# Channel attention and a SiLU feed-forward in fp32: factor sums of batch two moved to VectorE in step 0 and reloaded from DRAM, step 0 reordered, own tiles for step 0's outputs

## The chip, the cores and the metric

One core of one Trainium2 chip. The number is the device time of one execution in microseconds, for the kernel before as the median of 3 runs. A profile is of one execution of its own.

## The reference, cut to what matters

```python
def _attn_ref(q, k, v, tau):            # (2, 6016, 256) each
    qn = q / (np.linalg.norm(q, axis=1, keepdims=True) + 1e-06)
    kn = k / (np.linalg.norm(k, axis=1, keepdims=True) + 1e-06)
    s = kn.transpose(0, 2, 1) @ qn / tau            # 256 x 256 per batch
    s = s - s.max(-1, keepdims=True)
    a = np.exp(s)
    a /= a.sum(-1, keepdims=True) + 1e-09
    return v @ a

def _moe_ref(x, w_in, w_out):           # x (12032, 256), w_in (256, 2048)
    h = x @ w_in
    g = h * (1.0 / (1.0 + np.exp(-h)))
    return g @ w_out
```

## The kernel before, in words

A first stage (to about 97 us) reads q and k, forms the 256 x 256 attention matrix of both batches and folds each into w_in, so that each batch has its own first-layer weight (`wp_raw[b]`). What is left is silu(v @ folded weight) @ w_out over 12032 tokens, in fp32 written as a high and a low fp32r part: each product is three matmuls (high by high, high by low, low by high). Both layers are done in 2x2 blocks with seven products in place of eight (a Strassen form). The seven weight factors of the first layer are three raw blocks (A12, A22, A11) and four sums (S1 to S4). They are called `a_hi`/`a_lo` here.

The tokens go through in 12 steps (6 for each batch, the last of each narrow, 448 columns in place of 512), and a step goes through 8 pairs of blocks of the hidden dimension. A period n is one pair of one step, n = 8 * step + pair, 96 in all. TensorE does in each the seven products p1 ... p7 of the first layer (lines 823 to 825, 21 matmuls), and the second layer for the period before. In step 0 (periods 0 to 7) that second layer is the plain one of eight products (24 matmuls, `output`, lines 870 to 874), and the Strassen one (21 matmuls, lines 883 to 885, weights from the double buffer `ring`, loaded from `s_dram`) takes over at period 9. While step 0 runs, the eight "parts" of the second layer's factors are made: SyncE loads w_out, GpSimd makes sums and high parts (`part`), VectorE the low parts (`split_part`), SyncE stores to `s_dram`. Parts 4 to 7 share one tile, `late_parts`, so that part i+1 is loaded only when part i is stored.

Each engine's order is written out by hand, in program order, with semaphores between the engines. In a period VectorE's two adds make_c22 (line 1558) and make_c21 (line 1567) stand on the chain of that period: the product p7 ends, make_c22 adds, ScalarE applies SiLU and rounds, VectorE subtracts to the low part (`split_h`, line 1572), and TensorE reads it in the next period. Everything else of VectorE is fitted around it.

At the switch of batches (periods 40 to 55) the first-layer factors of batch two take the places of batch one's, pair by pair. In the kernel before, SyncE reloads the raw blocks (`load_a1`), GpSimd makes four sums with six subtractions and two casts (`prepare_a1`), VectorE makes the low parts (`split_a1`, lines 1546 and 1548):

```python
        reload_at = {SWITCH + 1 + 3 * pair // 2 + pair // 6: pair for pair in range(PAIRS)}
```

The tokens of a step (`load_x`, 6 DMAs on SyncE's queue, then 5 adding DMAs on GpSimd's) go through the tile `x_raw`, rounded by ScalarE (`round_x`) and split by VectorE (`split_x`). In the kernel before, step 0's four outputs are copied into `x_raw`, stored from there, and only then are the tokens of step 2 loaded:

```python
            store_std_outputs()
            sp.wait_ge(out_stored, 32)
            load_x(2)
```

SyncE's queue around it: ring loads for periods 8 and 9 (the second waits for the end of period 8 on TensorE), store part 5, load part 6, then the lines above.

## Time and profile before

| | us |
|---|---|
| median of 3 runs | 1074.22 (1074.03 to 1078.78) |
| profiled execution | 1070.89 |
| its span | 1069.1 |
| TensorE busy | 1034.2 (97%) |
| VectorE busy | 934.1 (87%) |
| ScalarE busy | 898.7 (84%) |
| GpSimd busy | 297.6 (28%) |

The profile gives one engine's busy time as the union of its instructions. Instructions of one engine overlap a little, so that one of 0.69 us can follow another by 0.60 us. The idle time in front of an instruction is printed in brackets with what ended it. A period starts at the first matmul of p1 (a row of L823).

### The profile page before, as it was taken

The page shows a single profiled execution, that of the slowest core. Times are in us where ns is not written, and L with a number is a line of the kernel's source. Part 1 is how long each engine was busy: PE and PEld are TensorE (multiplying, and loading weights), DVE is VectorE, ACT ScalarE, POOL GpSimd, SP SyncE. Part 2 cuts the span into 40 slices and gives each one's busy share as a digit, 9 for nine tenths or more (in the row PEclk, how much of TensorE's full clock was granted, in tenths as well). Part 3 has the DMA queues.
Part 4 walks back from the last instruction along what each step waited for, and adds up shares of the span by engine and source line. Part 5 has one row for each costly group of instructions (what it writes and reads, how often), then busy time and mean ns, then how long its engine had stood idle before and what let it go on. Part 6 is the DMA issues. An engine that isn't in the chain of part 4 may idle for free.

```text
span 1069.1 us, 15160 instructions
## 1 busy us (share of the span) xinstructions
PE 1034.2 (97%) x4584; PEld 851.6 (80%) x4584; DVE 934.1 (87%) x1307; ACT 898.7 (84%) x1580; POOL 297.6 (28%) x323
## 2 busy tenths in 40 slices
PE   9999998989999999999978999999999999999997
PEld 8987776767888888888867777888888888888886
DVE  6887685689889899899899999899899899899898
ACT  7997676778898998898867788898898898988875
POOL 3695231143120121221273662121121211210100
PEclk9999999999999999999999999999999999999999
DMA  9993421397786885876975885885876876975742
GB/s 358 397 366 89 151 92 66 133 265 176 199 194 152 215 196 135 216 176 148 255 150 143 225 193 124 219 188 132 235 173 152 217 173 147 229 168 130 176 134 88
DMA packets 107921, 197.06 MB, mean 184 GB/s; under 512 B 9424, under 2 KB 42448, under 8 KB 107712
## 3 DMA queue, kind: packets, MB, share of 16 engines
q1 hardware_dynamic: 82720, 150.07, 43.2%
q0 software_dynamic: 24544, 45.17, 25.9%
q8 instruction: 37, 0.61, 0.2%
q10 hardware_dynamic: 576, 0.85, 0.2%
q14 instruction: 44, 0.36, 0.1%
HBM read 145.82 MB, written 50.23 MB: 183 GB/s over the span
## 4 chain that ended last, share of the span: by engine, by line
PE 71%; DVE 6%; ACT 3%; issue 3%; DMA 2%; SPq 1%; DVEq 0%; POOL 0%; ACTq 0%; POOLq 0%
PE ps_h L823 12%; PE ps_h L825 12%; PE ps_h L824 12%; PE ps_o L883 6%; PE ps_o L884 6%; PE ps_o L885 6%; PE ps_h L883 5%; PE ps_h L885 5%; PE ps_h L884 5%; DVE t_raw L1584 1%; DVE g_lo L1572 1%; DMA ring<-s_dram 1%; PE ps_o L870 1%; PE ps_o L872 1%; PE ps_o L874 1%
## 5 line engine op out<-in xcount | busy, mean ns | idle before, releaser
L1572 DVE TENSOR_TENSOR g_lo<-h,g_hi 128x512 fp32r<-128x512 f32 (+1 forms) x296 | 205.4, 696 | 24.5 <-ACT g_hi L1206 23.2
L1206 ACT ACTIVATE g_hi<-h 128x512 fp32r<-128x512 f32 (+1 forms) x296 | 182.5, 620 | 10.2 <-PE ps_h L885 3.8
...
L823 PE MATMUL ps_h<-b_hi,a_hi_mid 128*128 128x512 f32 (+1 forms) x336 | 132.7, 395 | 6.1 <-ACT h L1183 3.1
L825 PE MATMUL ps_h<-b_hi,a_lo_mid 128*128 128x512 f32 (+1 forms) x336 | 130.9, 390 | 0.0
L824 PE MATMUL ps_h<-b_lo,a_hi_mid 128*128 128x512 f32 (+1 forms) x336 | 130.7, 389 | 0.0
L1558 DVE TENSOR_TENSOR h<-ps_h,w 128x512 f32<-128x512 f32 (+1 forms) x96 | 65.2, 679 | 61.5 <-PE ps_h L825 41.7
L883 PE MATMUL ps_h<-g_hi,ring 128*128 128x512 f32 (+1 forms) x264 | 103.7, 393 | 13.5 <-DVE g_lo L1572 7.2
L1606 DVE TENSOR_TENSOR gx_lo<-t_raw,gx_hi 128x1024 fp32r<-128x1024 f32 (+1 forms) x88 | 107.8, 1225 | 0.6 <-ACT gx_hi L1213 0.6
L1584 DVE TENSOR_TENSOR t_raw<-h 128x1024 f32<-128x1024 f32 (+1 forms) x88 | 107.4, 1221 | 0.0
L883 PE MATMUL ps_o<-gx_hi,ring 128*128 128x512 f32 (+1 forms) x264 | 102.2, 387 | 0.7 <-DVE gx_lo L1616 0.4
L885 PE MATMUL ps_h<-g_hi,ring 128*128 128x512 f32 (+1 forms) x264 | 102.7, 389 | 0.0
L884 PE MATMUL ps_h<-g_lo,ring 128*128 128x512 f32 (+1 forms) x264 | 102.5, 388 | 0.0
L884 PE MATMUL ps_o<-gx_lo,ring 128*128 128x512 f32 (+1 forms) x264 | 102.0, 386 | 0.0
L885 PE MATMUL ps_o<-gx_hi,ring 128*128 128x512 f32 (+1 forms) x264 | 102.0, 386 | 0.0
L1234 ACT ACTIVATE fl_sb<-ps_h 128x512 f32<-128x512 f32 (+1 forms) x81 | 48.0, 593 | 51.9 <-PE ps_h L885 42.4
L1213 ACT ACTIVATE gx_hi<-t_raw 128x1024 fp32r<-128x1024 f32 (+1 forms) x88 | 90.4, 1028 | 1.4 <-PE ps_o L885 0.7
L823 PEld LDWEIGHTS ps_h<-b_hi,a_hi_mid 128*128 128x128 f32 x336 | 63.5, 189 | 27.3 <-ACT h L1183 5.5
L1171 ACT ACTIVATE u<-ps_h 128x512 f32<-128x512 f32 (+1 forms) x96 | 56.7, 590 | 23.8 <-PE ps_h L825 21.4
L1449 DVE TENSOR_TENSOR square_sum<-ps_h,square_sum 128x768 f32<-128x768 f32 (+2 forms) x66 | 57.5, 912 | 18.3 <-ACT ps_h L1067 17.1
L825 PEld LDWEIGHTS ps_h<-b_hi,a_lo_mid 128*128 128x128 f32 x336 | 63.6, 189 | 12.4
L883 PEld LDWEIGHTS ps_h<-g_hi,ring 128*128 128x128 f32 x264 | 49.9, 189 | 29.3 <-issue 13.7
...
## 6 DMA issues: line engine op xcount, KB each, us to landing
...
```

What stands on the lines that cost most here:

```text
L823: nc.tensor.matmul(out, w_hi, x_hi, start=start, stop=False, skip_group_check=True)
L824: nc.tensor.matmul(out, w_hi, x_lo, start=False, stop=False, skip_group_check=True)
L825: return nc.tensor.matmul(out, w_lo, x_hi, start=False, stop=True, skip_group_check=True)
L883: nc.tensor.matmul(out[:, 0:tok], w_hi, x_hi[:, 0:tok], start=start, stop=False, skip_group_check=True)
L884: nc.tensor.matmul(out[:, 0:tok], w_hi, x_lo[:, 0:tok], start=False, stop=False, skip_group_check=True)
L885: return nc.tensor.matmul(out[:, 0:tok], w_lo, x_hi[:, 0:tok], start=False, stop=True, skip_group_check=True)
L1206: nc.scalar.activation(g_hi[:, g, 0:tok], h[:, g, 0:tok], ACT.Copy).then_inc(hi[g], 1)
L1213: nc.scalar.activation(gx_hi[:, GT1:GT3 + 1, 0:tok], t13_raw[:, :, 0:tok], ACT.Copy).then_inc(t13_hi, 1)
L1558: nc.vector.tensor_tensor(h[:, H22, 0:tok], ps_h[:, BANK_Y, 0:tok], w[:, 0:tok], ALU.add).then_inc(c22_made, 1)
L1572: nc.vector.tensor_tensor(g_lo[:, g, 0:tok], h[:, g, 0:tok], g_hi[:, g, 0:tok].bitcast(F32), ALU.subtract).then_inc(lo[g], 1)
L1584: nc.vector.tensor_tensor(t13_raw[:, :, 0:tok], h[:, H11:H12 + 1, 0:tok], h[:, H12:H22 + 1, 0:tok], ALU.add).then_inc(t13_made, 1)
L1606: nc.vector.tensor_tensor(gx_lo[:, GT1:GT3 + 1, 0:tok], t13_raw[:, :, 0:tok], gx_hi[:, GT1:GT3 + 1, 0:tok].bitcast(F32), ALU.subtract).the ...
```

## The change

It does this:

- VectorE makes the sums of batch two's factors for all eight pairs at once, in periods 1 and 2, out of `wp_raw[1]` (four instructions of 128x1024). ScalarE's queue stores raw blocks and sums to DRAM with four DMAs. At the switch SyncE loads all seven factors of a pair straight into `a_lo(pair)`, ScalarE rounds them into `a_hi` (128x896), and VectorE subtracts in place (one 128x896). GpSimd has nothing to do there.
- In step 0 VectorE's extra work (split_a, parts, tokens) goes behind the two splits that open a period and ahead of make_c22, or between make_c22 and the next split. Parts 6 and 7 are split in halves in periods 9 and 11, in place of whole ones in 10 and 12.
- Step 0's outputs get tiles of their own (`fl`, `u_sum` and two new ones), stored by four DMAs, and `load_x(2)` no longer waits for them. Later steps' tokens are loaded one period later.
- The probabilities of batch two have their own high part, rounded two copies earlier.

```diff
-        reload_at = {SWITCH + 1 + 3 * pair // 2 + pair // 6: pair for pair in range(PAIRS)}
+        A1_SPLIT_AT = (42, 44, 46, 48, 49, 50, 52, 54)
+        a1_split_at = {n: pair for pair, n in enumerate(A1_SPLIT_AT)}
+        a1_load_at = {max(n - 2, SWITCH + 1): pair for pair, n in enumerate(A1_SPLIT_AT)}
...
             def load_a1(pair):
-                sp.wait_ge(a_split, PAIRS)
-                if pair >= 2:
-                    sp.wait_ge(a1_split, pair - 1)
-                sp.dma_start(a1_raw[pair % 2][:], a1_dram[:, pair]).then_inc(a1_loaded[pair % 2], 16)
+                sp.wait_ge(a1_saved, 64)
+                sp.wait_ge(p4_done, SWITCH + pair + 1)
+                sp.dma_start(a_lo(pair).bitcast(F32), a1_dram[:, pair]).then_inc(a1_loaded[pair % 2], 16)
...
             load_part(6)
-            store_std_outputs()
-            sp.wait_ge(out_stored, 32)
+            sp.wait_ge(x_split, x_groups(1))
             load_x(2)
+            for t, c in ((1, 0), (1, 1), (0, 0), (0, 1)):
+                store_std_output(t, c)
...
-            def prepare_a1(pair):
...
                 round_h(n, TOK, H11, silu_11)
+                if n == 1:
+                    act.wait_ge(a1_step, 2)
+                    act.dma_start(a1_dram[:, :, A12:A11 + 1], wp_raw[1][:, :, 0:3, :]).then_inc(a1_saved, 16)
+                    act.dma_start(a1_dram[:, :, S3], wp_raw[1][:, :, 3, :]).then_inc(a1_saved, 16)
+                if n == 2:
+                    act.wait_ge(a1_step, 4)
+                    act.dma_start(a1_dram[:, :, S1:S2 + 1], a1_sums[:, :, 0:2, :]).then_inc(a1_saved, 16)
+                    act.dma_start(a1_dram[:, :, S4], a1_sums[:, :, 2, :]).then_inc(a1_saved, 16)
...
+            def round_a1(pair):
+                act.wait_ge(a1_loaded[pair % 2], 16 * (pair // 2 + 1))
+                nc.scalar.activation(a_hi(pair), a_lo(pair).bitcast(F32), ACT.Copy).then_inc(a1_rounded, 1)
...
+                if n + 1 in a1_split_at:
+                    round_a1(a1_split_at[n + 1])
...
             def flush(n):
                 tok = width(n)
                 act.wait_ge(used[H21], n + 1)
                 if n > FIRST:
                     act.wait_ge(fl_stored, 16 * (n - FIRST))
+                else:
+                    act.wait_ge(out_stored[0], 16)
...
+            def sum_a1_first():
+
+                dve.wait_ge(wp_copied, 2 * FOLDS)
+                a12, a22, a11, a21 = (wp_raw[1][:, :, i, :] for i in range(4))
+                nc.vector.tensor_tensor(a1_sums[:, :, 0, :], a22, a21, ALU.subtract).then_inc(a1_step, 1)
+                dve.wait_ge(a1_step, 1)
+                nc.vector.tensor_tensor(a21, a11, a21, ALU.subtract).then_inc(a1_step, 1)
...
             def split_a1(pair):
                 dve.wait_ge(a1_rounded, pair + 1)
-                nc.vector.tensor_tensor(a_lo(pair)[:, 0:3, :], a1_raw[pair % 2][:, 0:3, :], a_hi(pair)[:, 0:3, :].bitcast(F32),
-                                        ALU.subtract)
-                nc.vector.tensor_tensor(a_lo(pair)[:, 3:7, :], a1_sums[pair % 2][:], a_hi(pair)[:, 3:7, :].bitcast(F32),
+                nc.vector.tensor_tensor(a_lo(pair), a_lo(pair).bitcast(F32), a_hi(pair).bitcast(F32),
                                         ALU.subtract).then_inc(a1_split, 1)
...
-            PARTS_AT = {1: 0, 2: 1, 3: 2, 4: 3, 6: 4, 8: 5, 10: 6, 12: 7}
+            PARTS_EARLY = {2: 1, 3: 2, 6: 4}
+            PARTS_LATE = {1: 0, 3: 3, 7: 5}
+            PARTS_AT = {FIRST + 1: 6, FIRST + 3: 7}
...
                 sum_t2(n - 1, before)
                 split_h(n - 1, before, H21)
+                if n in PARTS_AT:
+                    split_part_raw(PARTS_AT[n])
...
                 sum_t4(n - 1, before)
                 split_t13(n - 1, before)
                 split_t4(n - 1, before)
+                if n in PARTS_AT:
+                    split_part_sums(PARTS_AT[n])
...
+                if n in a1_split_at:
+                    split_a1(a1_split_at[n])
                 make_c22(n, tok)
```

VectorE's order from the turn to the second layer's Strassen form, before: make_c22 and make_c21 of period 8, the split of part 5 (`late_parts`), then period 9 from its line 1594 (sum_t2).

```order
L1558 TENSOR_TENSOR h<-ps_h,w 128x512
L1567 TENSOR_TENSOR h<-ps_h,u 128x512
L1584 TENSOR_TENSOR t_raw<-h 128x1024
L1572 TENSOR_TENSOR g_lo<-h,g_hi 128x512 x2
L1540 TENSOR_TENSOR late_parts<-late_parts 128x512
L1541 TENSOR_TENSOR late_parts<-late_parts 128x384
L1594 TENSOR_TENSOR t_raw<-t_raw,h 128x512
L1572 TENSOR_TENSOR g_lo<-h,g_hi 128x512
L1601 TENSOR_TENSOR h<-t_raw,h 128x512
L1606 TENSOR_TENSOR gx_lo<-t_raw,gx_hi 128x1024
L1616 TENSOR_TENSOR gx_lo<-h,gx_hi 128x512
L1558 TENSOR_TENSOR h<-ps_h,w 128x512
```

The same stretch of VectorE now (line numbers of the changed kernel, L1569 is make_c22, L1605 sum_t2, L1528 and L1532 the halves of a part, here part 6):

```order
L1569 TENSOR_TENSOR h<-ps_h,w 128x512
L1578 TENSOR_TENSOR h<-ps_h,u 128x512
L1595 TENSOR_TENSOR t_raw<-h 128x1024
L1583 TENSOR_TENSOR g_lo<-h,g_hi 128x512 x2
L1605 TENSOR_TENSOR t_raw<-t_raw,h 128x512
L1583 TENSOR_TENSOR g_lo<-h,g_hi 128x512
L1528 TENSOR_TENSOR late_parts<-late_parts 128x512
L1612 TENSOR_TENSOR h<-t_raw,h 128x512
L1617 TENSOR_TENSOR gx_lo<-t_raw,gx_hi 128x1024
L1627 TENSOR_TENSOR gx_lo<-h,gx_hi 128x512
L1532 TENSOR_TENSOR late_parts<-late_parts 128x384
L1569 TENSOR_TENSOR h<-ps_h,w 128x512
```

Part 5 has left this stretch (it is split in period 7 now), and part 6, which stood in period 10, stands in period 9, its first half in front of sum_t4 (L1612).

VectorE in period 42, the first with a split of batch two's factors, before: from sum_u (L1634) on.

```order
L1634 TENSOR_TENSOR u_sum_sb<-ps_o,o_sb 128x512
L1601 TENSOR_TENSOR h<-t_raw,h 128x448
L1606 TENSOR_TENSOR gx_lo<-t_raw,gx_hi 128x2x448
L1616 TENSOR_TENSOR gx_lo<-h,gx_hi 128x448
L1558 TENSOR_TENSOR h<-ps_h,w 128x448
L1572 TENSOR_TENSOR g_lo<-h,g_hi 128x448
L1611 TENSOR_TENSOR g_lo<-t_raw,g_hi 128x448
L1567 TENSOR_TENSOR h<-ps_h,u 128x448
L1546 TENSOR_TENSOR a_lo_first<-a_raw,a_hi_first 128x384
L1548 TENSOR_TENSOR a_lo_first<-sums,a_hi_first 128x512
L1584 TENSOR_TENSOR t_raw<-h 128x2x448
```

And now, from the same sum_u (L1647):

```order
L1647 TENSOR_TENSOR u_sum_sb<-ps_o,o_sb 128x512
L1612 TENSOR_TENSOR h<-t_raw,h 128x448
L1617 TENSOR_TENSOR gx_lo<-t_raw,gx_hi 128x2x448
L1627 TENSOR_TENSOR gx_lo<-h,gx_hi 128x448
L1559 TENSOR_TENSOR a_lo_first<-a_lo_first,a_hi_first 128x896
L1569 TENSOR_TENSOR h<-ps_h,w 128x448
L1583 TENSOR_TENSOR g_lo<-h,g_hi 128x448
L1622 TENSOR_TENSOR g_lo<-t_raw,g_hi 128x448
L1578 TENSOR_TENSOR h<-ps_h,u 128x448
L1595 TENSOR_TENSOR t_raw<-h 128x2x448
```

The split of the factors was two instructions behind make_c21 and is one in front of make_c22.

## Rows read from the trace of the kernel before

**Rows 1.** Windows: length; busy us (x) of PE, PEld, DVE, ACT, POOL; clock, DMA

```profile
135.71:146.05 10.34, 10.34 (x47) 8.38 (x45) 8.09 (x15) 8.29 (x15) 2.80 (x6) 1.00 0.31 114
146.05:194.10 48.05, 43.61 (x181) 34.55 (x180) 30.68 (x52) 30.81 (x54) 11.04 (x17) 0.96 0.22 75
204.56:239.99 35.43, 30.21 (x122) 23.21 (x120) 29.99 (x42) 26.50 (x47) 10.91 (x12) 0.95 0.86 254
443.82:501.56 57.74, 57.74 (x253) 47.28 (x252) 53.48 (x77) 52.13 (x94) 10.18 (x12) 1.00 0.72 171
520.26:595.50 75.24, 65.37 (x295) 55.09 (x294) 70.75 (x96) 56.33 (x108) 39.25 (x53) 0.98 0.70 171
595.50:668.98 73.48, 69.02 (x295) 54.15 (x294) 70.56 (x96) 61.65 (x110) 34.38 (x40) 1.00 0.74 179
995.79:1047.82 52.03, 52.03 (x253) 46.60 (x252) 46.42 (x75) 43.19 (x83) 4.35 (x5) 1.00 0.55 142
```

**Rows 2.** Timeline of TensorE at the start of period 6

```profile
170.20 0.75 PE L823 MATMUL ps_h<-b_hi,a_hi_last 128*128 128x512 f32 x1 [2.10 <-DVE a_lo_last L1519]
173.96 0.39 PE L823 MATMUL ps_h<-b_hi,a_hi_last 128*128 128x512 f32 x1
```

**Rows 3.** Timeline of step 0, VectorE ahead of make_c22, and ScalarE in period 4

```profile
121.34 0.69 DVE L1558 TENSOR_TENSOR h<-ps_h,w 128x512 f32<-128x512 f32 x1 [3.14 <-PE ps_h L825]
131.83 0.69 DVE L1558 TENSOR_TENSOR h<-ps_h,w 128x512 f32<-128x512 f32 x1 [1.42 <-PE ps_h L825]
...
152.15 0.60 ACT L1183 ACTIVATE h<-ps_h 128x512 f32<-128x512 f32 x1 [2.28 <-DVE g_lo L1572]
```

**Rows 4.** Groups by shape, whole span: 128x1024 on VectorE, 128x896 on ScalarE

```profile
L1496 DVE TENSOR_TENSOR wo_lo<-wo_raw,wo_hi 128x1024 fp32r<-128x1024 f32 x4 | 4.7, 1218 | 0.0
...
L1213 ACT ACTIVATE gx_hi<-t_raw 128x896 fp32r<-128x896 f32 x16 | 15.1, 942 | 0.0
```

**Rows 5.** Timeline of period 10: the load of step 2's tokens

```profile
217.24 2.73 SPq L400 DMA_DIRECT2D x_raw<-v_t_dram  x6
...
224.95 1.15 ACT L1153 ACTIVATE b_hi<-x_raw 128x512 fp32r<-128x512 f32 x2 [3.65 <-DMA x_raw<-v_t_dram]
...
228.00 0.55 PE L883 MATMUL ps_h<-g_hi,ring 128*128 128x512 f32 x1 [3.42 <-DVE h L1567]
```

**Rows 6.** Timeline around periods 8 to 10: ring load, store of part 5, load of part 6, and its readers

```profile
205.36 0.61 SPq L427 DMA_DIRECT2D ring<-s_dram  x1
207.53 0.33 SPq L413 DMA_DIRECT2D s_dram<-late_parts  x1
...
212.10 0.33 SPq L407 DMA_DIRECT2D late_parts<-w_out_dram  x1
...
208.02 0.69 DVE L1572 TENSOR_TENSOR g_lo<-h,g_hi 128x512 fp32r<-128x512 f32 x1
...
210.71 0.50 PE L823 MATMUL ps_h<-b_hi,a_hi_first 128*128 128x512 f32 x1 [1.04 <-ACT h L1183]
...
214.69 1.15 POOL L630 TENSOR_TENSOR late_parts<-late_parts 128x128 f32<-128x128 f32 x1 [18.47 <-DMA late_parts<-w_out_dram]
...
219.42 1.50 POOL L638 CAST late_parts<-late_parts 128x384 fp32r<-128x384 f32 x1
```

**Rows 7.** Timeline of GpSimd, first and last instruction of part 0

```profile
117.82 0.69 POOL L630 TENSOR_TENSOR parts<-parts 128x128 f32<-128x128 f32 x1 [18.30 <-DMA parts<-w_out_dram]
...
120.63 0.51 POOL L638 CAST parts<-parts 128x384 fp32r<-128x384 f32 x1
```

**Rows 8.** VectorE's add L1584, 128x896: period 42's, mean in 530:660, in 1000:1050; ScalarE's DMA issue

```profile
540.31 3.12 DVE L1584 TENSOR_TENSOR t_raw<-h 128x896 f32<-128x896 f32 x1
...
L1584 DVE TENSOR_TENSOR t_raw<-h 128x896 f32<-128x896 f32 x6 | 8.5, 1420 | 0.0
...
L1584 DVE TENSOR_TENSOR t_raw<-h 128x896 f32<-128x896 f32 x6 | 6.5, 1081 | 0.0
...
0.74 0.89 ACTq L1387 DMA_DIRECT2D qk<-k_dram  x2
```

More of the change, by code:

```diff
@@ L133, in channel_attention_ffn @@
         sums = sb("sums", [P, 4, P])
-        a1_sums = [sums, sums1]
         x_raw = sb("x_raw", [P, 6, TOK])
-        out_sb = x_raw[:, 0:4, :].rearrange("p (t c) n -> p t c n", c=CK)
         b_hi = [sb("b_hi0", [P, FACTORS, TOK], F32R)]
@@ L149, in channel_attention_ffn @@
             w_in_lo = sb("w_in_lo", [P, CK, F], F32R, stack=early)
-            probs_hi = sb("probs_hi", [P, CK, C], F32R, stack=early)
+            probs_hi = [sb(f"probs_hi{b}", [P, CK, C], F32R, stack=early) for b in range(B)]
             probs_lo = sb("probs_lo", [P, CK, C], F32R, stack=early)
@@ L166, in channel_attention_ffn @@
         a_lo_last = sb("a_lo_last", [P, EARLY, FACTORS, P], F32R)
+        with ExitStack() as early:
+            a1_sums = sb("a1_sums", [P, PAIRS, 3, P], stack=early)
         b_hi += [sb("b_hi1", [P, FACTORS, TOK], F32R)]
@@ L348, in width @@
             return tokens_of(n // PAIRS)[1]
[L351 to L352 removed]
+        A1_SPLIT_AT = (42, 44, 46, 48, 49, 50, 52, 54)
+        a1_split_at = {n: pair for pair, n in enumerate(A1_SPLIT_AT)}
+        a1_load_at = {max(n - 2, SWITCH + 1): pair for pair, n in enumerate(A1_SPLIT_AT)}
+        assert SWITCH == 40 and all(SWITCH + pair < n for n, pair in a1_load_at.items())
+        assert all(n < SWITCH + PAIRS + pair for n, pair in a1_split_at.items())
         X_FIRST = ((T1, T2), (T3, T3), (B11, B22), (T4, T4))
[L356 to L357 removed]
+        X_LATER = (B11, T2, B21, T1, B22, T3, T4)
         def x_groups(step):
@@ L813, in fold @@
                 for j in range(CK):
-                    nc.tensor.matmul(out, probs_hi[:, j, c], w_in_hi[:, j, f], start=(j == 0), stop=False)
-                    nc.tensor.matmul(out, probs_hi[:, j, c], w_in_lo[:, j, f], start=False, stop=False)
+                    nc.tensor.matmul(out, probs_hi[b][:, j, c], w_in_hi[:, j, f], start=(j == 0), stop=False)
+                    nc.tensor.matmul(out, probs_hi[b][:, j, c], w_in_lo[:, j, f], start=False, stop=False)
                     mm = nc.tensor.matmul(out, probs_lo[:, j, c], w_in_hi[:, j, f], start=False, stop=(j == CK - 1))
@@ L1702, in pair_step @@
                 split_t4(n - 1, before)
+                if n in PARTS_AT:
+                    split_part_sums(PARTS_AT[n])
+                if it > 1 and pair == 0:
+                    split_x(it, T4, T4)
                 if it < FINAL:
```

156 lines of the change are left out of this document (70 added, 86 removed).

## The prediction

> **What bounds the kernel now.** I read the windows first, cut at the starts of periods. In the quiet middle (443.82 to 501.56, six wide periods) TensorE is busy for all 57.74 us, 9.62 us a period or 0.228 us a matmul, while VectorE is busy for 93% and ScalarE for 90%; six narrow periods near the end take 52.03 us, 8.67 each [rows 1]. These are TensorE's own pace, and no edit off TensorE can shorten them. What can be won is the excess over this pace, and it lies in three places:
>
> - Periods 4 to 7: 48.05 us, where four periods like period 3 (10.34 us, TensorE busy throughout) take 41.36. Excess 6.7 us [rows 1].
> - Periods 9 to 11: 35.43 us. Period 9 has 36 matmuls, so the pace is 8.2 + 9.62 + 9.62 = 27.5. Excess 7.9 us [rows 1].
> - Periods 41 to 54: 75.24 + 73.48 = 148.7 us, where seven narrow and seven wide ones take 7 x 8.67 + 7 x 9.62 = 128.0. Excess 20.7 us [rows 1].
>
> Then I read the timeline at each for what the excess is. TensorE stops 2.10 us in front of period 6 for `a_lo_last`, and its next nine matmuls start over 3.76 us (170.20 to 173.96) where the pace gives 2.05: the granted clock is 0.96 in this window, and so a stop of 2.1 us costs 3.8 [rows 1, 2]. In period 4 ScalarE's SiLU waits 2.28 us for VectorE's low part [rows 3], which stood behind token and part work. In period 10 ScalarE waits 3.65 us for the tokens of step 2, issued at 217.24 behind the stores, and TensorE stops 3.42 us [rows 5].
>
> **The switch.** VectorE is busy there for 70.75 + 70.56 = 141.3 us over 192 instructions. At the mean of the quiet windows (46.42/75 = 0.619 narrow, 53.48/77 = 0.695 wide) 96 + 96 of them would take 126.1 [rows 1]. So 15.2 us of VectorE's time is stretching. One add of 128x896 took 3.12 us; its mean is 1.42 there and 1.08 at the end of the kernel [rows 8]. GpSimd is busy 39.25 + 34.38 us in these windows and 10 in the quiet one [rows 1]. The Trainium skill, "SBUF — State Buffer", section "SBUF: two separate sides", says that VectorE with two SBUF inputs and GpSimd take turns on one port pair under a lock, and that DMA traffic does not slow either. The rows agree with the first half.
>
> The change takes all of GpSimd's work out of the switch. VectorE keeps its splits (one 128x896 in place of two pieces), so it has about 126 us of work in 128.0 us of TensorE's pace, 98%, where the quiet middle has 93%. It won't all come back. Bounds: with no residue 20.7 us. With each of the eight splits, now ahead of make_c22, landing whole on the chain at 1.08 us less its overlap, about 1.0 us [rows 8], 20.7 - 8 = 12.7. Only some of these periods also carry a token split or sum_u in front of make_c22, and make_c22 has TensorE's line of two products behind p7 as cover (1.4 us at the pace); if that cover were gone the residue would be the 8 us. I take a residue of 3.7: **gain 17**. ScalarE gets eight roundings of 0.94 us [rows 4]; it is busy 56.33 + 61.65 of 148.7 us now [rows 1], so of 128 it would have 118 + 7.5 = 125.5, 98% too, which is why I don't take less residue. SyncE's new loads wait for p4 of a period that has ended before the ring load behind them is due: cost 0.
>
> **Step 0.** Parts, tokens and split_a move behind the opening splits and ahead of make_c22, into idle time of VectorE of 3.14 us in period 1, 1.42 in period 2 [rows 3]. The stops of periods 4 to 7 go: 6.7 us, of which I leave 0.3. Added are four instructions of 128x1024 at 1.22 us [rows 4]. In period 1, 2.4 us go into 3.14 idle: hidden, were GpSimd not at part 0 from 117.82 to 121.14 [rows 7]; say 0.5. In period 2, 2.4 us and part 1's split stand ahead of make_c22, 3.5 us into 1.42 idle plus the 1.1 that part 0 leaves: 1.0 late, and all of it on the chain. ScalarE's two DMA issues of 0.45 us each (0.89 for two) [rows 8] in periods 1 and 2 delay its next copy: 0.25 each. Sum 2.0, between 0 (all hidden) and 4 (stretched by GpSimd too). **Net gain 4.4**, from 2.4 to 6.4. The earlier rounding of the probabilities gives at most some tenths, as VectorE's sums stand before it: 0.
>
> **Part six.** This is what I think speaks most against the change. Part 6's first half stands in period 9 now, ahead of sum_t4. It needs GpSimd's part 6, that needs load_part(6), that the store of part 5, and that stands in SyncE's queue behind the second ring load, which waits for the end of period 8. None of this queue moved. Before, the ring loads end at 205.97, the store goes at 207.53 (it waited for VectorE), the next load at 212.10, 4.57 us on, and GpSimd starts 2.59 us later [rows 6]. Now the store is ready and goes at 205.97, so the load at 210.5, GpSimd at 213.1. Alone it takes 3.3 us for a part (117.82 to 121.14 [rows 7]), beside a working VectorE 6.2 (214.69 to 220.92 [rows 6]); VectorE waits, so 3.3, done at 216.4. VectorE arrives when its split of H21 is through: at 208.70 before [rows 6], less 1.1 for part 5, at 207.6. It waits 8.8 us. Behind it queue sum_t4, then ScalarE's rounding of it, then SiLU of c11, for which TensorE holds p7. Before, p7 went at 210.71 [rows 6]; sum_t4 would be through at 217.7, rounding and SiLU take 1.1, so p7 at 219.0: 8.3 later. By [rows 2] the low clock behind a stop adds some 1.4 (3.8 for 2.1 leaves 1.7). So period 9 costs 9.7 more. The tokens (load at 211.4 to 214.1, landing by about 219) are there for period 10, which is later too, and the new wait of the first flush for the store out of `fl` (third store, about 219) is covered by the same stop. Without that stop the flush would wait some 3 us. So of the old excess of 7.9 in periods 9 to 11 the part of period 10's stop goes, 3.42 us [rows 5] and some 1.9 of low clock behind it: 5.3. Part 7 in period 11 hangs on the store behind the ring load of period 10: from that period's start 0.7 + 4.57 + 2.59 + 3.3 = 11.2 us, with 6.2 for GpSimd 14.1, and VectorE gets there some 3 us into period 11, at 12.6; I take 1.0. **Net loss 9.7 - 5.3 + 1.0 = 5.4**, between 3 (chain 1 us shorter, part of the wait covered) and 10 (GpSimd at its slow 6.2, 1.7 at part 7).
>
> Later steps: the same work, tokens loaded a period later but read a period later too; TensorE is never idle in the quiet window [rows 1]: 0. Small stops in period 13 and 17: 0.4 gained.
>
> **Sum**: 17 + 4.4 - 5.4 + 0.4 = 16.4 us. Against its own execution 1070.9 (span 1069.1 and 1.8 around it) this is 1054.5. The median of the runs is 3.3 above the profiled one, so **1057.8**.
>
> **Rivals.**
>
> 1. *Part six's wait does not reach TensorE* (the load lands early or the chain has more room than I see): then also the excess of periods 9 to 11 goes. 17 + 4.4 + 7.9 + 0.4 = 29.7, 1044.5. For it: VectorE has some slack. Against: the queue order and 8.8 us of wait. 7%.
> 2. *The switch stays bound*, VectorE and ScalarE at 98% with the split ahead of make_c22: residue 12.7 rather than 3.7. 16.4 - 9 = 7.4 gained, 1066.8. For it: in the quiet windows VectorE is never above 93%. 15%.
> 3. *Slower: the stretching is not GpSimd's but the DMA's* that write SBUF. Then nothing comes back at the switch, and eight roundings of 0.94 us less overlap, 6.7 us, land on ScalarE's chain: -6.7 + 4.4 - 5.4 + 0.4 = 7.3 slower, 1081.5. It decides if less than 1 us comes back. Against: the DMA share is 0.72 in the quiet middle and 0.70 and 0.74 at the switch [rows 1], with no stretching in the first. By the Trainium skill, the same section, DMAs can't do this at all, and the trace agrees. 4%.
>
> My forecast has the remaining 74%. I keep 1049 to 1067: errors of 3 to 4 us in each of the three big terms, and the better half of rival 2. Outside lie rivals 1 and 3, half of rival 2 and the forecast's tails, 20% together. Within 0.5% (5.4 us, about what a measurement of this kernel tells from nothing) needs a gain below 5.4: 6%, from the end of rival 2. Slower by more: 4%. Faster by more: 90%.
>
> **What the profile after would show.** Right: at the switch VectorE's L1595 of 128x896 at 1.08 us mean and TensorE stopping for less than 2 us there; TensorE idle for 7 to 9 us in period 9 at an L823-like product of the first layer, with VectorE's L1528 (`late_parts`) waiting for GpSimd's cast and the clock low after it; no wait of ScalarE for `x_raw` in period 10; no stop for `a_lo_last`. Wrong: VectorE reaching L1528 of period 9 with GpSimd done; VectorE's adds at the switch still over 1.3 us; or ScalarE without idle time in periods 42 to 54 and TensorE stopping in most of them.

## The result: 1107 us, 3% slower than before

The changed kernel takes 1107.05 us (median of 4 runs, 1103.38 to 1112.46), beside 1074.5 us for the kernel before (4 runs in this round). The ratio is 1.030, 95% interval 1.024 to 1.036. The prediction was 1057.8 us, 1049 to 1067: wrong in size and in sign. The profiled execution took 1103.89 us, span 1102.1; that of before 1070.9 and 1069.1, so the two traces differ by 33.0 us.

The windows of the changed kernel, cut at the starts of the same periods as in [rows 1] (periods 4 to 7, 9 to 11, 33 to 38, 41 to 47, 48 to 54):

```profile
core 0: us, PE busy (x) PEld busy (x) DVE busy (x) ACT busy (x) POOL busy (x), PEclk, DMA share, GB/s
150.08:192.93 42.85, 41.52 (x182) 33.38 (x181) 29.37 (x53) 31.84 (x55) 8.40 (x13) 1.00 0.19 62
203.19:248.54 45.35, 30.54 (x121) 23.92 (x120) 27.43 (x39) 26.22 (x47) 10.97 (x18) 0.85 0.72 206
459.15:521.69 62.54, 59.56 (x254) 48.31 (x253) 52.62 (x75) 52.02 (x93) 12.83 (x15) 0.97 0.74 175
540.38:611.54 71.16, 63.83 (x296) 55.18 (x294) 58.00 (x90) 59.01 (x112) 13.67 (x16) 0.98 0.82 211
611.54:684.50 72.96, 68.78 (x296) 54.49 (x294) 64.80 (x92) 63.89 (x113) 13.70 (x16) 1.00 0.76 188
```

Beside [rows 1]: periods 4 to 7 are 5.2 us shorter, the switch 4.6 us (144.1 for 148.7), periods 9 to 11 are 9.9 us longer. The surprise is the third row. That was the quiet middle, where TensorE was never idle; it is 4.8 us longer now, and TensorE is idle for 3 us in it. The chain of the page says where to look. Its first line gives the shares by engine (71% PE and 2% DMA before), the second those by line:

```profile
PE 62%; DMA 15%; ACT 10%; issue 4%; DVE 4%; POOL 4%; SPq 1%; ACTq 0%; DVEq 0%; POOLq 0%
PE ps_h L796 11%; PE ps_h L798 10%; PE ps_h L797 10%; DMA out_t_dram<-fl_sb 8%; PE ps_o L856 5%; PE ps_o L857 5%; PE ps_o L858 5%; PE ps_h L856 4%; PE ps_h L857 4%; PE ps_h L858 4%; ACT ps_h L1040 3%; DMA out_t_dram<-o_sb 3%; DMA s_dram<-la
```

8% of the span hangs on the store out of `fl`, which the chain of before did not list among its leading lines. Cut by periods, the trace shows one long period in each of steps 2 to 10, always pair 3 (periods 19, 27, ... 83): 13.76, 14.36, 14.42, 15.67, 13.86, 12.83, 15.06, 16.49 and 12.21 us. Over 9.6 us each that is 42.3 us; the same nine periods had 5.6 over it before (4.5 of them in period 43, at the switch). TensorE stops there for 30.2 us in all. Period 27 in the timelines, GpSimd's queue first, then ScalarE and TensorE, in the changed kernel:

```profile
387.73 0.87 POOL L658 DMA_DIRECT2D out_t_dram<-o_sb  x1 [8.23 <-DMA out_t_dram<-o_sb]
388.27 1.22 POOL L652 DMA_DIRECT2D out_t_dram<-o_sb  x1
388.81 3.37 POOL L603 DMA_DIRECT2D x_raw<-v_t_dram  x3
390.43 2.32 POOL L647 DMA_DIRECT2D out_t_dram<-fl_sb  x1
400.23 0.60 ACT L1210 ACTIVATE fl_sb<-ps_h 128x512 f32<-128x512 f32 x1 [3.91 <-DMA out_t_dram<-fl_sb]
401.88 0.50 PE L796 MATMUL ps_h<-b_hi,a_hi_mid 128*128 128x512 f32 x1 [2.90 <-ACT ps_h L1141]
402.22 0.39 PE L797 MATMUL ps_h<-b_lo,a_hi_mid 128*128 128x512 f32 x1
402.82 0.63 PE L796 MATMUL ps_h<-b_hi,a_hi_mid 128*128 128x512 f32 x1
403.25 0.63 PE L797 MATMUL ps_h<-b_lo,a_hi_mid 128*128 128x512 f32 x1
```

and in the kernel before, the rows that answer to these:

```profile
378.42 1.58 POOL L606 DMA_DIRECT2D x_raw<-v_t_dram  x1
378.96 1.61 POOL L650 DMA_DIRECT2D out_t_dram<-fl_sb  x1
386.55 0.60 ACT L1234 ACTIVATE fl_sb<-ps_h 128x512 f32<-128x512 f32 x1 [0.83 <-DMA out_t_dram<-fl_sb]
```

`fl` is one tile. ScalarE's flush of a pair copies a finished sum from `ps_h` into it, and GpSimd issues the DMA that adds it to the output in DRAM, the store out of `fl`. So the flush of a pair waits until the store of the pair before has landed. In pair 2 of a step that store is issued late, since GpSimd first waits 8.2 us for an earlier store to the output block c21, and then issues in program order what has become due. Before, one adding token load stood ahead of it; now there are three. From the start of period 26 (376.40 before, 387.24 after) the store has landed, and the flush starts, 10.15 us on in the one and 12.99 us in the other: 0.6 us of later issue, 2.2 us of longer flight. The period lasts 9.6 us, so 0.8 us of wait became 3.9, ScalarE's `seed_u1` behind it is late, and TensorE stops 2.90 us for that. From 402.82 to 405.81 it then starts its matmuls 0.43 us apart instead of 0.228, and the clock granted in this stretch is 0.50 (1.2 of 2.4 GHz): a stop of 2.9 us costs 4.8.

The other stretch that grew, period 9 (23.36 us):

```profile
204.64 0.60 SPq L415 DMA_DIRECT2D s_dram<-late_parts  x1
211.89 0.33 SPq L409 DMA_DIRECT2D late_parts<-w_out_dram  x1
214.40 0.45 POOL L627 TENSOR_TENSOR late_parts<-late_parts 128x128 f32<-128x128 f32 x1 [25.93 <-DMA late_parts<-w_out_dram]
216.95 0.51 POOL L635 CAST late_parts<-late_parts 128x384 fp32r<-128x384 f32 x1
217.49 0.69 DVE L1528 TENSOR_TENSOR late_parts<-late_parts 128x512 fp32r<-128x512 f32 x1 [11.23 <-POOL late_parts L635]
218.81 0.63 ACT L1201 ACTIVATE gx_hi<-h 128x512 fp32r<-128x512 f32 x1 [11.96 <-DVE h L1612]
219.98 0.79 PE L796 MATMUL ps_h<-b_hi,a_hi_first 128*128 128x512 f32 x1 [11.70 <-ACT h L1157]
```

This is the chain that the prediction drew, link by link, but its first link is 7.25 us (store to next load) and not 4.57 as in [rows 6].

### The profile page after: what moved, and what is told of

Same layout as the page of the kernel before. It is cut to its first block, busy times and chain, and to the rows that moved or that the text cites. A ratio compares the mean times of both kernels' runs of the same rounds, so it can differ in the third digit from the quotient of the medians.

```text
span 1102.1 us, 15090 instructions
## 1 busy us (share of the span) xinstructions
PE 1040.5 (94%) x4584; PEld 857.6 (78%) x4584; DVE 920.4 (84%) x1303; ACT 905.8 (82%) x1588; POOL 244.1 (22%) x259
## 4 chain that ended last, share of the span: by engine, by line
PE 62%; DMA 15%; ACT 10%; issue 4%; DVE 4%; POOL 4%; SPq 1%; ACTq 0%; DVEq 0%; POOLq 0%
PE ps_h L796 11%; PE ps_h L798 10%; PE ps_h L797 10%; DMA out_t_dram<-fl_sb 8%; PE ps_o L856 5%; PE ps_o L857 5%; PE ps_o L858 5%; PE ps_h L856 4%; PE ps_h L857 4%; PE ps_h L858 4%; ACT ps_h L1040 3%; DMA out_t_dram<-o_sb 3%; DMA s_dram<-late_parts 1%; DVE square_sum L1436 1%; DMA s_dram<-parts 1%
## 5 line engine op out<-in xcount | busy, mean ns | idle before, releaser
L1583 DVE TENSOR_TENSOR g_lo<-h,g_hi 128x512 fp32r<-128x512 f32 (+1 forms) x296 | 200.9, 681 | 53.2 <-ACT g_hi L1180 51.7
L796 PE MATMUL ps_h<-b_hi,a_hi_mid 128*128 128x512 f32 (+1 forms) x336 | 135.0, 402 | 32.1 <-ACT ps_h L1141 29.3
L1569 DVE TENSOR_TENSOR h<-ps_h,w 128x512 f32<-128x512 f32 (+1 forms) x96 | 65.2, 679 | 57.3 <-PE ps_h L798 47.3
L1617 DVE TENSOR_TENSOR gx_lo<-t_raw,gx_hi 128x1024 fp32r<-128x1024 f32 (+1 forms) x88 | 105.5, 1199 | 0.2 <-ACT gx_hi L1187 0.2
L1595 DVE TENSOR_TENSOR t_raw<-h 128x1024 f32<-128x1024 f32 (+1 forms) x88 | 104.9, 1192 | 0.0
L796 PE MATMUL ps_h<-b_hi,a_hi_first 128*128 128x512 f32 (+1 forms) x168 | 67.0, 399 | 11.7 <-ACT h L1157 11.7
L603 POOL DMA_DIRECT2D x_raw<-v_t_dram x55 | 58.0, 1475 | 73.9 <-DMA x_raw<-v_t_dram 55.9
```

Of the source, the lines that this page charges most:

```text
L796: nc.tensor.matmul(out, w_hi, x_hi, start=start, stop=False, skip_group_check=True)
L1583: nc.vector.tensor_tensor(g_lo[:, g, 0:tok], h[:, g, 0:tok], g_hi[:, g, 0:tok].bitcast(F32), ALU.subtract).then_inc(lo[g], 1)
L1595: nc.vector.tensor_tensor(t13_raw[:, :, 0:tok], h[:, H11:H12 + 1, 0:tok], h[:, H12:H22 + 1, 0:tok], ALU.add).then_inc(t13_made, 1)
L1617: nc.vector.tensor_tensor(gx_lo[:, GT1:GT3 + 1, 0:tok], t13_raw[:, :, 0:tok], gx_hi[:, GT1:GT3 + 1, 0:tok].bitcast(F32), ALU.subtract).the ...
```

## The experiments

All ratios are to the kernel before, run on the same chip. The experiments were made in three rounds on three chips, and the kernel before took 1075.75 us beside e1 to e4, 1074.99 beside e5, e6, e8 and e9, and 1072.87 beside e10 and e11. Where two kernels of different rounds are compared, the ratios tell more than the medians. The table gives the lengths of stretches of each profiled execution in us, each the difference between the starts of TensorE's first product of two periods. The column pair 3 is the sum over 9.6 us of the nine periods named above; those of steps 5 and 6 also lie in the switch.

| kernel | median | ratio (95%) | periods 2-8 | 9-11 | 41-54 | pair 3 |
|---|---|---|---|---|---|---|
| before | 1074.5 | 1 | 79.3 | 35.4 | 148.7 | 5.6 |
| changed | 1107.05 | 1.030 (1.024 to 1.036) | 76.9 | 45.4 | 144.1 | 42.3 |
| e1, old tokens | 1070.55 | 0.995 (0.993 to 0.998) | 78.7 | 49.1 | 138.4 | 5.6 |
| e2, new tokens alone | 1106.77 | 1.028 (1.023 to 1.033) | 78.0 | 37.8 | 154.7 | 42.9 |
| e3, loads behind the flush | 1081.86 | 1.004 (1.002 to 1.007) | 77.2 | 50.1 | 141.0 | 10.6 |
| e4, parts back | 1102.53 | 1.025 (1.019 to 1.030) | 76.9 | 40.6 | 145.6 | 43.9 |
| e5, e1 and e4 | 1066.38 | 0.992 (0.990 to 0.995) | 76.9 | 40.8 | 138.6 | 2.0 |
| e8, e5 and early store | 1062.0 | 0.988 (0.985 to 0.991) | 76.7 | 39.1 | 137.9 | 2.5 |
| e6, e8 and busy GpSimd | 1076.76 | 1.002 (1.000 to 1.004) | 77.0 | 40.1 | 152.9 | 8.4 |
| e9, e1 with later adding loads | 1107.57 | 1.030 (1.027 to 1.033) | 77.3 | 46.6 | 143.4 | 40.0 |
| e10, e8 and first flush ahead | 1057.45 | 0.984 (0.981 to 0.987) | 76.8 | 33.0 | 137.9 | 7.5 |
| e11, e10 and saves by SyncE | 1053.92 | 0.981 (0.979 to 0.983) | 75.5 | 31.9 | 137.6 | 3.8 |

The column 9-11 is of one execution each, and it varies. Up to period 15 e3 has the instructions and DMAs of the changed kernel in the same order, and yet its periods 9 to 11 take 50.1 us for 45.4. The difference lies in period 11, 17.57 us long where the changed kernel has 12.44 (16.91 in e1, 13.23 in e9). The load of part 7 follows the store of part 6 there after 10.56 us (7.42 in the changed kernel), and VectorE waits 5.60 us for part 7 and not 2.98. The rows of e3:

```profile
224.44 0.61 SPq L416 DMA_DIRECT2D s_dram<-late_parts  x1
235.00 0.33 SPq L410 DMA_DIRECT2D late_parts<-w_out_dram  x1
240.88 0.69 DVE L1539 TENSOR_TENSOR late_parts<-late_parts 128x512 fp32r<-128x512 f32 x1 [5.60 <-POOL late_parts L640]
```

### Whose are the stops of pair 3: e1 and e2

e1 puts the whole token schedule of before into the changed kernel. Its core:

```diff
-                if pair == 0 and it + 1 < ALL:
-                    sp.wait_ge(x_split, x_groups(it))
-                    load_x(it + 1)
                 load_ring_b(n)
+                if pair == PAIRS - 1 and it + 2 < ALL:
+                    sp.wait_ge(x_split, x_groups(it + 1))
+                    load_x(it + 2)
...
-                if it > 1 and pair == 1 and it + 1 < ALL:
+                if it > 1 and pair == 0 and it + 1 < ALL:
                     add_x_first(it + 1)
-                if pair == 2 and it + 1 < ALL:
+                if pair == (1 if it > 1 else 3) and it + 1 < ALL:
                     add_x_second(it + 1)
```

> The changed kernel with the whole token schedule of the kernel before put back: SyncE's six loads at the end of the step, GpSimd's three adding loads in pair 0 and the fourth in pair 1, the old order of roundings and splits. Nothing of the computation is left out. My theory now: the token schedule alone makes the stop of 2.3 to 4.6 us in pair 3 of steps 2 to 10 (nine periods of 12.2 to 16.5 us that took 9.6 before, some 43 us in all). It then gives 1107 - 43 = 1064 us, TensorE does not stop in period 27 and the flush there waits under 1 us. Rival: the slower pair 3 comes from another part (the flush's own tile, the outputs' new tiles, GpSimd's load): then it stays above 1095 us. Period 9 keeps its stop of 11 to 12 us in either case.

1070.55 us: 36.5 less than the changed kernel, and 6.5 above my 1064. The pair 3 column falls by 36.7 to its value of before. ScalarE's flush in period 27 still waits 1.25 us, where I expected less than 1, and TensorE stops for 0.44 us, not for nothing.

e2 is the kernel before with the opposite of this edit, from step 3's tokens on.

> The kernel before with the new token schedule alone, from step 3's tokens on. Nothing is left out. My theory: the stops of pair 3 appear without any other part of the change, in steps 2 to 9 or 10: 1074 + 40 = 1114 us, with period 27 at 13 to 15 us. Rival: they need the rest of the change too: within 5 us of 1074.

1106.77 us, 31 more than the kernel before in this round and 7 below my 1114; period 27 takes 14.3 us and the pair 3 column is 42.9: the stops need nothing else of the change. The token schedule alone accounts for as much as the whole result, because the rest of the change gains little on balance.

### Queue order or transfer load: e9 and e3

Two things of the token schedule moved: SyncE's six loads into pair 0, and GpSimd's adding loads one pair later. e9 keeps the first in its old place and moves only the second, with the roundings and splits of the old step 2 so that they come after the later loads:

```diff
-                if it > 1 and pair == 0 and it + 1 < ALL:
+                if it > 1 and pair == 1 and it + 1 < ALL:
                     add_x_first(it + 1)
-                if pair == (1 if it > 1 else 3) and it + 1 < ALL:
+                if pair == (2 if it > 1 else 3) and it + 1 < ALL:
                     add_x_second(it + 1)
```

> The changed kernel with the old token schedule, except that GpSimd's adding loads stand one pair later (three in pair 1, right ahead of the flush's store, the fourth in pair 2, the last in pair 6), with roundings and splits in the order of the old step 2; SyncE's six loads stay in their old place, at the end of the step before. Theory A (the place of GpSimd's three loads ahead of the flush's store in its queue makes the stop): the stops of pair 3 are back, 1070.5 + 30 = 1100 us or more. Theory B (SyncE's six loads in pair 0 make it): no stops, within 6 us of 1070.5.

1107.57 us, 37.0 above e1 (1.030 for 0.995), and pair 3 has 40.0. Its timeline at period 27:

```profile
387.85 3.37 POOL L604 DMA_DIRECT2D x_raw<-v_t_dram  x3
389.48 2.32 POOL L648 DMA_DIRECT2D out_t_dram<-fl_sb  x1
400.23 0.60 ACT L1211 ACTIVATE fl_sb<-ps_h 128x512 f32<-128x512 f32 x1 [3.47 <-DMA out_t_dram<-fl_sb]
```

The same picture with SyncE's loads elsewhere: theory B falls. e3 is the other way round. SyncE's loads stay in pair 0 as changed, one adding load stays in pair 1, and two go behind the flush's store of the next period:

```diff
-                add_x(step, X_T2, 0, 1).then_inc(t_first, 16)
+                add_x(step, X_T2, 0, 1).then_inc(t_two, 16)
+                if step < 3:
+                    add_x_rest(step)
+
+            def add_x_rest(step):
                 add_x(step, X_T1, 0, 1).then_inc(t_first, 16)
                 add_x(step, X_T3, 1, 1).then_inc(t_first, 16)
...
                 if pair == 2 and it + 1 < ALL:
                     add_x_second(it + 1)
+                    if it > 1:
+                        add_x_rest(it + 1)
```

> The changed kernel, where from step 3's tokens on only one of the three adding loads goes in pair 1, and the other two go behind the flush of pair 2 and the fourth adding load in GpSimd's queue. SyncE's six loads stay in pair 0 as changed; bytes and issues are the same. Theory A (order in GpSimd's DMA queue: the store out of fl stands behind three adding loads of 256 KB, which put its landing some 3 us later): most of the 43 us comes back, 1070 to 1080 us, and the flush of period 27 waits under 2 us. Theory B (the six loads on SyncE in pair 0 load the DMA engines, and everything that lands then lands late): the stops of pair 3 stay, over 1095 us. Theory C (too many bytes for one period, wherever they stand): the stop moves to pair 4 with about its size, over 1090 us.

1081.86 us: 25 of the 36.5 us come back; pair 3 falls to 10.6. In period 27 the queue and the flush now read:

```profile
387.39 1.57 POOL L604 DMA_DIRECT2D x_raw<-v_t_dram  x1
387.93 1.59 POOL L652 DMA_DIRECT2D out_t_dram<-fl_sb  x1
396.11 0.60 ACT L1221 ACTIVATE fl_sb<-ps_h 128x512 f32<-128x512 f32 x1 [0.80 <-DMA out_t_dram<-fl_sb]
```

The median is 2 us above the range of theory A. What stays has two parts: the pair after it, where three loads are now ahead of the next store (period 28 takes 10.5 us, period 60 11.5), which is theory C in small; and VectorE and ScalarE in steps 8 to 10 (period 75 12.3 us, TensorE stopping 1.98 us for VectorE's `h`), whose cause I did not separate. So bytes, loads, SyncE's place and the order of the roundings and splits are the same in e3 as in the changed kernel, and the order in GpSimd's queue alone decides two thirds. The Trainium skill, "DMA: Bandwidth & Descriptors", section "Queues, rings and completion order", says of the queues of SyncE and ScalarE that each DMA engine takes descriptors in the order of the ring. The traces here fit such an order in GpSimd's queue too: the store lands later when two more loads are ahead of it (12.99 against 10.15 us).

### What stands behind part six: e4, e5, e8, e10

e4 puts parts 6 and 7 back into periods 10 and 12, behind make_c21, and SyncE's store and load with them:

```diff
-            PARTS_AT = {FIRST + 1: 6, FIRST + 3: 7}
+            PARTS_AT = {FIRST + 2: 6, FIRST + 4: 7}
...
-                if n == FIRST + 2:
+                if n == FIRST + 3:
                     store_part(6)
```

> The changed kernel with parts 6 and 7 split whole in periods 10 and 12, behind make_c21, as before the change, and SyncE's store of part 6 and load of part 7 back in their old places. Nothing is left out. Periods 9 to 11 have 17.9 us over TensorE's pace in the changed kernel. My theory: VectorE's wait of 11.2 us for GpSimd's part 6 goes, and with it the stop of TensorE in period 9 (11.7 us); under it comes up the first flush's wait for the first store out of fl, some 3 us; so 7 to 11 us less than the changed kernel: 1096 to 1100. Rival: the stop belongs to the tokens of step 2 or to the stores and only changes its name: less than 4 us gained.

1102.53 us, 4.5 less; 2.5 us above my range, and near the rival's 4. In the trace the rival is right about what happened: the stop of period 9 is gone (9.85 us), and period 10 takes 20.7 us. SyncE, ScalarE and TensorE there:

```profile
213.82 0.66 SPq L434 DMA_DIRECT2D out_t_dram<-fl_sb  x1
220.31 0.60 ACT L1210 ACTIVATE fl_sb<-ps_h 128x512 f32<-128x512 f32 x1 [10.41 <-DMA out_t_dram<-fl_sb]
221.97 0.79 PE L796 MATMUL ps_h<-b_hi,a_hi_mid 128*128 128x512 f32 x1 [9.43 <-ACT ps_h L1141]
```

The first flush waits for the store of step 0's output out of `fl`, which SyncE issues third of four, behind part 5's store, the wait for it, part 6's load and the six token loads. The prediction gave this wait 3 us. It is 10.4, and it was hidden under part 6's.

e5 is e4's edit on e1.

> The changed kernel with the old token schedule and parts 6 and 7 back in periods 10 and 12: of the change stay the sums by VectorE, step 0's order and the outputs' own tiles. Nothing is left out. With parts back alone, TensorE's stop only moved from period 9 (11.7 us) to period 10 (9.4 us, the first flush waiting 10.4 us for the store out of fl, which SyncE issues behind part 5's store, its wait and six token loads). My theory: the same here, but the six token loads stand there in this kernel too, so period 10 still stops 8 to 10 us; against the old tokens alone (1070.5) it gains what parts back gained (4.5 us): 1064 to 1067 us. Rival: with the tokens' order back the store is early enough: 1056 to 1059 us.

1066.38 us, within my range (3 us below e1 by the ratios), and period 10 takes 20.73 us with 9.3 of stop: the rival falls. e8 adds one move in SyncE's queue:

```diff
             store_part(5)
+            store_std_output(0, 0)
             sp.wait_ge(part_stored, part_stored_by(5))
...
-            for t, c in ((1, 0), (1, 1), (0, 0), (0, 1)):
+            for t, c in ((1, 0), (1, 1), (0, 1)):
```

> The kernel above, where SyncE issues the store out of fl right behind the store of part 5, ahead of its wait and of the six token loads (10 us earlier). Nothing is left out. My theory: the second reason for the stop in periods 9 and 10 was this store; its wait goes, and periods 9 to 11 fall to about 30 us from 40.6: 1053 to 1057 us. Rival: a third wait stands behind it (the tokens of step 2, as in period 10 of the kernel before, 3.4 us of stop): 1058 to 1062 us.

1062.0 us, the top of the rival's range, 5 us above mine. The flush's wait in period 10 is gone (20.73 to 12.08 us), but period 11 takes 17.2 us:

```profile
220.38 2.67 POOL L605 DMA_DIRECT2D x_raw<-v_t_dram  x3 [1.85 <-DMA x_raw<-v_t_dram]
222.04 1.58 POOL L649 DMA_DIRECT2D out_t_dram<-fl_sb  x1
230.47 0.60 ACT L1212 ACTIVATE fl_sb<-ps_h 128x512 f32<-128x512 f32 x1 [6.64 <-DMA out_t_dram<-fl_sb]
232.13 0.79 PE L798 MATMUL ps_h<-b_hi,a_hi_mid 128*128 128x512 f32 x1 [5.13 <-ACT ps_h L1143]
```

The third wait is neither my theory nor the rival's tokens: it is the mechanism of pair 3 once more. GpSimd waits for the six token loads, issues three adding loads, and the first flush's store goes behind them. e10 turns that order:

```diff
-            add_x_first(2)
             for n in range(FIRST + 2, PERIODS):
...
+                if n == FIRST + 2:
+                    add_x_first(2)
```

> The kernel with the early store of fl, where GpSimd issues step 2's three adding loads behind the first flush's store instead of ahead of it. Nothing is left out. In the kernel with the early store, GpSimd waits for the six token loads to land until 220.38, issues three adding loads and the store out of fl behind them at 222.04; ScalarE's next flush waits 6.64 us for it and TensorE stops 5.1 us in period 11 (17.2 us). My theory: this is the same mechanism as the stop of pair 3 in the later steps, and with the order turned the store goes at about 213 us and period 11 takes 10 to 11 us: 1062.0 - 6.5 = 1055.5 us. Rival: the tokens of step 2 come too late instead (roundings of them in ScalarE in periods 10 and 11 wait), and less than 3 us come back.

1057.45 us, 4.6 less by the medians and 4.0 by the ratios (I expected 6.5); periods 9 to 11 fall from 39.1 to 33.0, by 6.1, and period 11 to 10.8. The store goes at 218.40, not at 213 as I wrote: GpSimd's part 6 stands ahead of it. Of the rival there is a rest in period 10: ScalarE waits 2.43 us for `x_raw`, and TensorE stops 2.1 us.

### The stretching of VectorE at the switch: e6

e6 is e8 with the amount of GpSimd work that the kernel before had at the switch, on a spare tile:

```diff
+                if n in reload_at:
+                    if reload_at[n] == 0:
+                        nc.gpsimd.memset(spare[:], 0.0).then_inc(spare_done, 1)
+                    for j in range(6):
+                        pool.wait_ge(spare_done, 8 * reload_at[n] + j + 1)
+                        nc.gpsimd.tensor_tensor(spare[:, 0, :], spare[:, 1, :], spare[:, 2, :],
+                                                ALU.subtract).then_inc(spare_done, 1)
...
```

> The kernel above plus GpSimd work on a spare tile at the switch (per factor pair six subtractions of 128x128 and two roundings, as the kernel before had, and one memset): work is added, the output is as before. It gives back GpSimd's load of VectorE's memory port and changes no transfer. My theory: VectorE's instructions in periods 41 to 54 stretch again, by 10 to 15 us in all, and the two windows of these periods, 138.4 us with the old tokens, come to 145 or more: 6 us or more above the kernel above. Rival (the stretching at the switch before was the DMA's, or GpSimd's work costs nothing): within 2 us of the kernel above.

1076.76 us, 14.8 above e8, and periods 41 to 54 take 152.9 for 137.9. The windows of periods 41 to 47 and 48 to 54, e6 first:

```profile
521.52:597.56 76.04, 66.60 (x295) 56.25 (x294) 66.60 (x91) 59.24 (x112) 42.36 (x54) 0.96 0.72 183
597.56:674.39 76.83, 71.43 (x296) 55.37 (x295) 70.51 (x93) 64.65 (x114) 35.14 (x40) 0.98 0.73 178
```

and e8:

```profile
521.82:588.91 67.09, 62.28 (x295) 53.97 (x294) 58.88 (x92) 58.48 (x112) 11.48 (x14) 1.00 0.81 204
588.91:659.74 70.83, 68.25 (x295) 54.62 (x294) 65.24 (x93) 64.39 (x114) 13.67 (x16) 1.00 0.78 197
```

VectorE is busy 137.1 us over 184 instructions beside a busy GpSimd and 124.1 over 185 without, with the same instructions: 13 us of stretching. The DMA share is the lower one in e6. So GpSimd's instructions make the stretching, not transfers. The Trainium skill, "SBUF — State Buffer", section "SBUF: two separate sides", gives the shared port pair of the two engines as the reason; that VectorE's busy time follows GpSimd's load and not the DMA's is what e6 shows of it.

The 15 us of time are not all due to this. In e6 the added work also stands ahead of a store out of `fl` in GpSimd's program. First e6, then e8, around the flush of period 43:

```profile
542.74 0.60 POOL L651 DMA_DIRECT2D out_t_dram<-fl_sb  x1
545.10 0.54 ACT L1225 ACTIVATE fl_sb<-ps_h 128x448 f32<-128x448 f32 x1 [5.08 <-DMA out_t_dram<-fl_sb]
```

```profile
542.80 0.55 ACT L1212 ACTIVATE fl_sb<-ps_h 128x448 f32<-128x448 f32 x1 [1.17 <-DMA out_t_dram<-fl_sb]
```

e8 issues this store at 535.68, and e6, whose period 42 starts at about the same time, at 542.74. TensorE stops behind the late flush (4.12 us for 0.45), and period 43 takes 15.43 us for 10.16; period 51 shows the same in small (11.52 for 10.25). These two periods are 6.5 of the 15 us. In others TensorE stops for VectorE (2.32 us in period 44, 2.41 in 52). So my sentence that the edit changes no transfer was not right, and how the 15 us divide between the late store and the stretching was not tried.

### Who issues the saves of step 0: e11

e11 lets SyncE issue the four saves, two ahead of part 0's store and two behind part 3's load.

```diff
-                if n == 2:
-                    act.wait_ge(a1_step, 4)
-                    act.dma_start(a1_dram[:, :, S1:S2 + 1], a1_sums[:, :, 0:2, :]).then_inc(a1_saved, 16)
...
+            sp.wait_ge(a1_step, 4)
+            sp.dma_start(a1_dram[:, :, S1:S2 + 1], a1_sums[:, :, 0:2, :]).then_inc(a1_saved, 16)
```

> The kernel above, where SyncE issues the four stores of batch two's factors and sums instead of ScalarE (two ahead of part 0's store, two behind part 3's load). Nothing is left out. ScalarE's issues took 0.58 and 1.37 us in period 1 and 0.52 and 0.74 in period 2, where periods 2 to 4 take 3.3 us more than before the change. Theory A: they lie beside ScalarE's waits for VectorE, which stands behind GpSimd's part 0 and is stretched by it; periods 2 to 4 stay within 0.7 us of their 35.5. Theory B (ScalarE's issues make its copies and SiLUs late): 1.5 us or more come back in periods 2 to 4.

1053.92 us. Periods 2 to 4 take 34.2 for 35.6: 1.4 us, between the two theories, and for a reason that neither names. Period 2, right behind ScalarE's first two issues, does not change (12.30 for 12.29 us); 1.0 of the 1.4 us comes in period 4, where ScalarE issues none. First e10, then e11:

```profile
144.90 0.46 POOL L629 TENSOR_TENSOR parts<-parts 128x128 f32<-128x128 f32 x1 [4.21 <-DMA parts<-w_out_dram]
148.01 0.69 DVE L1532 TENSOR_TENSOR parts<-parts 128x512 fp32r<-128x512 f32 x1 [2.27 <-POOL parts L637]
```

```profile
141.28 0.63 POOL L635 TENSOR_TENSOR parts<-parts 128x128 f32<-128x128 f32 x1 [1.31 <-DMA parts<-w_out_dram]
145.54 0.69 DVE L1530 TENSOR_TENSOR parts<-parts 128x512 fp32r<-128x512 f32 x1 [0.88 <-POOL parts L643]
```

With the saves issued ahead of it (by ScalarE, at 137.0 and 137.6), part 3's load, issued at 139.0, reaches GpSimd's first instruction 5.9 us later; with the saves behind it 2.7 us later (138.5 to 141.3), and VectorE waits 1.4 us less for GpSimd. The saves' price was in a transfer of another queue, not in ScalarE's issue time. The 3.5 us between the medians of e10 and e11 are more than this: e10's periods 19 and 35 are 1.3 and 1.6 us longer than e11's, without an edit there, and I can't say why.

## Why the prediction was wrong, step by step

**"Later steps: the same work, tokens loaded a period later but read a period later too"**, put at 0, is the step that failed. I asked of the moved loads only whether their data came in time, and not what they are queued ahead of. On GpSimd's queue they moved from behind one store of `fl` to right ahead of the next, in the one period of a step where that store is already late, since GpSimd waits 8 us for c21. The profile before had the row that should have warned: the flush in period 27 waited 0.83 us for that store, so there was no slack. And the quiet window from which I read "never idle" shows TensorE, not ScalarE's wait behind it. Measured: 42.3 - 5.6 = 36.7 us in nine periods (e1: 36.5 us on the medians; e2 and e9 bring it back each by itself). No rival was this one; the one on the slower side, that DMAs stretch VectorE, falls with e6.

**"The switch"**, gain 17 with a residue of 3.7. The mechanism was right: mean of VectorE's 128x896 adds there

```profile
L1595 DVE TENSOR_TENSOR t_raw<-h 128x896 f32<-128x896 f32 x8 | 8.7, 1082 | 0.0
```

for 1420 in [rows 8], and e6 brings 13 us of stretching back. The gain in the changed kernel is still only 4.6: periods 41 to 54 are 16.1 us over their pace of 128.0. Of these 11.2 stand in periods 43 and 51, which carry stops of pair 3 (7.0 and 4.2 us over their paces of 8.67 and 9.62). The other twelve periods have 4.9, of which 2.1 are in period 41, before the first split (TensorE stops 1.63 us for VectorE's `h`); that is a little above my 3.7. The split that now stands ahead of make_c22 costs less than the 1.0 us of my bound: periods 44 and 46 take 9.03 and 9.05 for 8.67, 52 and 54 take 9.88 and 9.89 for 9.62. It costs the whole 1.0 only with the old token schedule: in e1, e5, e8, e10 and e11 periods 41 to 54 take 137.6 to 138.6, 9.6 to 10.6 over the pace, with 9.65 in 44 and 46, 10.5 in 52 and 10.7 in 54. There VectorE has two token splits in front of the factor split in period 46, and one in the changed kernel; e4 and e9, with one, have 9.0 to 9.1 in 44 and 46 too. So the residue depends on what else the period of a split carries. With e1's 3.7 in periods 43 and 51 the changed kernel would have 8.6, a gain of 12 and not 17; no run shows it without its pair 3 stops and with its own order of tokens.

**"Step 0"**, net gain 4.4, between 2.4 and 6.4. Periods 2 to 8 went from 79.3 to 76.9: 2.4. Periods 5 to 7 gained 5.4 us and have no stop now. The stop of period 4, which I had counted as gone with them, is still there (1.33 us, the period 11.87 for 11.64), so it is 5.4 where I had 6.4. And what is added costs more than my 2.0: periods 2 to 4 are 3.2 us longer. In period 1 GpSimd's part 0 now takes 5.4 us (118.67 to 124.09) for 3.3 before; VectorE waits for it, and the instruction behind the waiting one, beside GpSimd's part 1, takes 1.50 us (0.55 for the same form in period 11):

```profile
124.12 0.69 DVE L1528 TENSOR_TENSOR parts<-parts 128x512 fp32r<-128x512 f32 x1 [0.88 <-POOL parts L635]
124.73 1.50 DVE L1532 TENSOR_TENSOR parts<-parts 128x384 fp32r<-128x384 f32 x1
128.69 0.50 PE L843 MATMUL ps_o<-g_hi,wo_hi 128*128 128x512 f32 x1 [1.58 <-DVE g_lo L1583]
```

That this makes period 2's stop is read from the trace and was not tried; e11 shows that ScalarE's issues do not. The "0.25 each" for these measured 1.4 together, through the transfers and in another place: 1.0 in period 4, 0.3 in period 3.

**"Part six"**, net loss 5.4, between 3 and 10; measured 9.9. The chain was right: VectorE waits 11.2 us (8.8 predicted) at L1528 for GpSimd's cast, TensorE stops 11.7 us (7 to 9 predicted) at the first layer's product, the granted clock is 0.50 in the 5 us behind it, period 10 has no stop and its tokens are covered. Period 9 is 12.4 us longer and not 9.7, period 10 is 4.1 shorter and not 5.3. The mis-sized term is the link from store to load, 7.25 us and not 4.57. Part 5's store follows the second ring load within 0.65 us now, where it was 1.6 us before; whether the ring's transfers ahead of it are the reason was not tried. Part 7 cost 1.7 and not 1.0 in this trace (period 11 12.44 us for 10.79) and 6.8 in e3, whose order of work is the same up to there. So it is partly luck that the 9.9 us lie in my range of 3 to 10: the same stretch of e3 is 14.6 us longer than before. And **"the new wait of the first flush", "some 3 us without that stop"**, was 10.4 (e4). So two waits of 10 to 11 us lay over each other, with a third, of 6.6, behind: removing the one I named would have been worth 4.5 us.

**"Small stops"**, 0.4: periods 12 to 15 gained 1.0.

The 33.0 us of the two traces: +1.1 ahead of period 2, -2.4 in 2 to 8, +9.9 in 9 to 11, -1.0 in 12 to 15, +12.5 in 16 to 40, -4.6 at the switch, +17.4 in 55 to 87 and +0.1 after.
